# One load per token tile, with gate factor and token number carried through the tiles, in a fused attention, MoE and gated-MLP kernel

## The reference, cut to what matters

```python
def reference(**kwargs):
    attn_out = _attn_ref(**attn_kwargs)          # recurrent attention, (B, H, S, D)
    x = attn_out.transpose(0, 2, 1, 3).reshape(B * S, H * D)
    x = _moe_ref(x=x, **moe_kwargs)
    return _moe2_ref(x=x, **moe2_kwargs)

def _moe_ref(x, w_gate, w_output_gate, w1, w2):
    logits = x @ w_gate
    e_idx = np.argmax(logits, axis=1)            # one expert for each token
    ...
    for e in range(E):
        mask = e_idx == e
        h = np.maximum(x[mask] @ w1[e], 0.0)
        ye = h @ w2[e]
        out[mask] = gate_w[mask, None] * eom[mask, e, None] * ye
    return out

def _moe2_ref(x, w_gate, w_val, w_out, rms_g):
    xn = x / np.sqrt(np.mean(x * x, axis=-1, keepdims=True) + 1e-06) * rms_g
    g = xn @ w_gate
    return (g / (1.0 + np.exp(-g)) * (xn @ w_val)) @ w_out
```

## Time and profile before

| what | value |
|---|---|
| median of 3 runs | 879.19 us (878.07 to 881.12) |
| profiled execution, its own time | 886.08 us |
| its span | 884.3 us |
| PE busy | 822.9 us (93%) |
| DVE busy | 511.9 us (58%) |
| ACT busy | 387.7 us (44%) |
| POOL busy | 135.9 us (15%) |
| q1, the queue that SP issues to | 103.11 MB, 42.2% of 16 engines |
| DMA packets | 92492, of them 19464 under 512 B |

### The profile page before, as it was taken

The page is one execution under the profiler, slowest core; times in us unless marked ns, Lnnn a source line. Parts: engine busy times, 40 slices in busy tenths (PEclk is TensorE's granted clock), DMA queues, the critical chain, the costliest instruction groups (busy, mean ns, idle before and its releaser), DMA issues.

```text
span 884.3 us, 18262 instructions
## 1 busy us (share of the span) xinstructions
PE 822.9 (93%) x6219; PEld 739.2 (84%) x6219; DVE 511.9 (58%) x1060; ACT 387.7 (44%) x703; POOL 135.9 (15%) x196
## 2 busy tenths in 40 slices
PE   7999999509999999999989999999999999999994
PEld 4877777408999999999988888888888888888884
DVE  5388877647687868777774354344344344344331
ACT  5454544115777777677673233233233233233221
POOL 3467776510000000000000001001001001001001
PEclk8699999657999999999999999999999999999998
DMA  5577775189999999998980100100100100100000
GB/s 184 131 185 205 198 201 154 64 249 269 267 265 264 282 272 280 258 278 254 300 231 16 37 1 30 37 1 30 36 0 30 36 0 30 36 0 30 1 1 30
DMA packets 92492, 114.30 MB, mean 129 GB/s; under 512 B 19464, under 2 KB 71208, under 8 KB 92440
## 3 DMA queue, kind: packets, MB, share of 16 engines
q1 hardware_dynamic: 87960, 103.11, 42.2%
q0 software_dynamic: 2304, 7.89, 2.6%
q10 hardware_dynamic: 2176, 2.64, 1.0%
HBM read 97.18 MB, written 16.46 MB: 129 GB/s over the span
## 4 chain that ended last, share of the span: by engine, by line
PE 71%; POOL 10%; issue 8%; DVE 3%; SPq 2%; DMA 2%; ACT 1%; ACTq 1%; POOLq 0%; DVEq 0%
PE psum L1459 41%; PE psum L1534 5%; PE psum L1533 5%; PE psum L1532 5%; PE psum L1486 4%; PE psum L1487 4%; PE psum L1488 3%; POOL zT L643 3%; POOL prob_T L617 2%; POOL x_by_expert L652 2%; DMA w_raw<-w 1%; POOL v_weighted L627 1%; PE psum L1451 1%; PE psum L1511 1%; PE psum L1372 1%
## 5 line engine op out<-in xcount | busy, mean ns | idle before, releaser
L1285 DVE TENSOR_TENSOR gated_lo<-gated,gated_hi 128x512 fp32r<-128x512 f32 x72 | 49.8, 692 | 181.5 <-ACT gated_hi L847 170.5
L842 ACT ACTIVATE sigm_sb<-psum 128x512 f32<-128x512 f32 x72 | 43.1, 598 | 248.9 <-PE psum L1459 234.1
L681 POOL DMA_INDIRECT out<-out_rows,slot_idx x24 | 23.0, 959 | 669.7 <-ACT out_rows L853 664.2
L1459 PE MATMUL psum<-nT_hi,w_gv_hi 128*128 128x512 f32 x432 | 122.2, 391 | 1.8 <-DVE nT_lo L1272 1.8
L1459 PE MATMUL psum<-nT_lo,w_gv_hi 128*128 128x512 f32 x432 | 121.9, 390 | 0.0
L1459 PEld LDWEIGHTS psum<-nT_lo,w_gv_hi 128*128 128x128 f32 x432 | 81.1, 188 | 17.8
L1459 PEld LDWEIGHTS psum<-nT_hi,w_gv_hi 128*128 128x128 f32 x432 | 78.6, 188 | 14.4 <-issue 2.1
L1532 PE MATMUL psum<-w_out_hi,gated_hi 128*128 128x320 f32 x288 | 89.1, 309 | 0.0
L1534 PE MATMUL psum<-w_out_hi,gated_lo 128*128 128x320 f32 x288 | 89.0, 309 | 0.0
L1533 PE MATMUL psum<-w_out_lo,gated_hi 128*128 128x320 f32 x288 | 88.9, 309 | 0.0
L1459 PE MATMUL psum<-nT_hi,w_gv_lo 128*128 128x512 f32 x288 | 88.7, 389 | 0.0
(11 more groups left out here) (206 smaller groups left out, 1564.1 us busy)
## 6 DMA issues: line engine op xcount, KB each, us to landing
w_raw<-w SPq DMA_DIRECT2D x38, 640.0 KB, 7.4
w_raw<-w SPq DMA_DIRECT2D x38, 512.0 KB, 4.8
w_raw<-w SPq DMA_DIRECT2D x76, 128.0 KB, 5.6
kv_tok<-tok SPq DMA_DIRECT2D x24, 324.0 KB
qk_sb<-qk SPq DMA_DIRECT2D x48, 160.0 KB
y_sorted<-y_tile SPq DMA_DIRECT2D x12, 321.0 KB, 5.4
og_tok<-o_tok SPq DMA_DIRECT2D x24, 160.0 KB
x_tile<-x_by_expert SPq DMA_DIRECT2D x12, 320.0 KB, 2.9
```

Source lines behind the costliest of these rows:

```text
L842: nc.scalar.activation(sigm_sb[f % 2][:], bank[2 * (f % 2)][:], ACT.Sigmoid).then_inc(sig_ready, 1)
L1285: dve.tensor_tensor(gated_lo[f % 4][:], gated[f % 2][:], gated_hi[f % 4][:].bitcast(F32), ALU.subtract).then_inc(hv_lo, 1)
L1459: m = mm(dst, w, x, start=(n == 0), stop=(n == len(terms) - 1))
```

## The change

The rows of `x_by_expert` become 386 columns wide (`XW`): 320, the last 64 again, gate factor, token number. ScalarE makes the 64 doubled columns in `y_tok` with a new function `double_tail`, 24 copies of 128 x 64 in the attention stage; each scatter waits for it. The zero rows are 386 columns wide too. `x_load` is one transfer of whole rows. In the expert stage GpSimd runs a new function `keep_meta(j)` for each tile: it copies the two extra columns from `x_tile` to a small buffer `row_meta`, and from there to `y_tile`, which is 323 columns wide now. The store writes all 323 columns, the copy from DRAM to DRAM and one table read are gone, `x_load(j)` waits for `meta_kept`, and the store waits for `meta_moved`.

```diff
             def x_load(j, w):
                 row = sp.value_load(rowi[0:1, bass.ds(j, 1)], min_val=0, max_val=IDLE)
                 wait(sp, xt_made, j)
-                xr = x_by_expert[bass.ds(row, w), :].rearrange("(s p) n -> p s n", p=P)
-                sp.dma_start(x_tile[:, 0:w // P, 0:DM], xr[:, :, 0:DM]).then_inc(x_in, 16)
-                sp.dma_start(x_tile[:, 0:w // P, DM:KB * P], xr[:, :, DM - TAIL:DM]).then_inc(x_in, 16)
+                wait(sp, meta_kept, j)
+                sp.dma_start(x_tile[:, 0:w // P], x_by_expert[bass.ds(row, w), :].rearrange("(s p) n -> p s n", p=P)).then_inc(x_in, 16)
...
             def expert_store(j, w):
-                row = sp.value_load(rowi[0:1, bass.ds(j, 1)], min_val=0, max_val=IDLE)
                 to = sp.value_load(stori[0:1, bass.ds(j, 1)], min_val=0, max_val=NTOK)
                 wait(sp, e_stored, 16 * j)
-                wait(sp, meta_in, 16 * j)
                 sp.sem_inc(sync_turn, 1)
-                sp.dma_start(y_sorted[bass.ds(to, w), DM + 1:YW], x_by_expert[bass.ds(row, w), DM:XW]).then_inc(meta_in, 16)
+                sp.wait_ge(meta_moved, j + 1)
+                sp.sem_inc(sync_turn, 1)
                 sp.wait_ge(e_copied, 2 * j + 2)
                 sp.wait_ge(e_squared, 2 * j + 2)
                 sp.sem_inc(sync_turn, 1)
-                sp.dma_start(y_sorted[bass.ds(to, w), 0:DM + 1].rearrange("(s p) n -> p s n", p=P), y_tile[:, 0:w // P]).then_inc(e_stored, 16)
+                sp.dma_start(y_sorted[bass.ds(to, w), :].rearrange("(s p) n -> p s n", p=P), y_tile[:, 0:w // P]).then_inc(e_stored, 16)
...
+            def keep_meta(j, w):
+                n = w // P
+                pool.wait_ge(x_in, 16 * j + 16)
+                pool.sem_inc(pool_turn, 1)
+                pool.tensor_copy(row_meta[:, 0:n], x_tile[:, 0:n, KB * P:XW]).then_inc(meta_kept, 1)
+                pool.wait_ge(meta_kept, j + 1)
+                pool.sem_inc(pool_turn, 1)
+                wait(pool, e_stored, 16 * j)
+                pool.sem_inc(pool_turn, 1)
+                pool.tensor_copy(y_tile[:, 0:n, DM + 1:YW], row_meta[:, 0:n]).then_inc(meta_moved, 1)
+                pool.wait_ge(meta_moved, j + 1)
+                pool.sem_inc(pool_turn, 1)
...
+            def double_tail(n):
+                act.wait_ge(y_ready, n + 1)
+                nc.scalar.activation(y_tok[:, n % NY, DM:KB * P], y_tok[:, n % NY, DM - TAIL:DM], ACT.Copy).then_inc(tail_doubled, 1)
...
                 if i + 3 < NT:
                     gates(i + 3)
+                if i >= 3:
+                    double_tail(i - 3)
```

More of the change, by code:

```diff
@@ L67 @@
 NY = 12
-XW = DM + 2
+XW = KB * P + 2
 YW = DM + 3
@@ L187, in build @@
         second_lo = sb("second_lo", [P, NF1, DM], F32R, ge)
-        x_tile = sb("x_tile", [P, 2, KB * P], F32, ge)
+        x_tile = sb("x_tile", [P, 2, XW], F32, ge)
         xT_hi = sb("xT_hi", [P, KB, TE], F32R, ge)
@@ L192, in build @@
         hT_lo = sb("hT_lo", [P, NF1 // 2, 2 * TE], F32R, ge)
-        y_tile = sb("y_tile", [P, 2, DM + 1], F32, ge)
+        y_tile = sb("y_tile", [P, 2, YW], F32, ge)
+        row_meta = sb("row_meta", [P, 2, 2], F32, ge)
         squares = sb("squares", [P, DM], F32, ge)
@@ L285, in build @@
         store_rows = sem("store_rows")
-        meta_in = sem("meta_in")
+        tail_doubled = sem("tail_doubled")
+        meta_kept = sem("meta_kept")
+        meta_moved = sem("meta_moved")
         cnt_table = sem("cnt_table")
@@ L533, in _ @@
             sp.wait_ge(e_stored, 16 * FIRST_STORES)
-            sp.wait_ge(meta_in, 16 * FIRST_STORES)
             c_load(0)
@@ L541, in _ @@
             sp.wait_ge(e_stored, 16 * NTE)
-            sp.wait_ge(meta_in, 16 * NTE)
             with sp.Fori(1, NTC) as t:
@@ L650, in scatter @@
                 pool.wait_ge(ids_made, n // B + 1)
+                pool.wait_ge(tail_doubled, n + 1)
                 pool.sem_inc(pool_turn, 1)
@@ L674, in _ @@
                 scatter(n)
+            def keep_meta(j, w):
[10 more added lines that the diff above has]
+                pool.sem_inc(pool_turn, 1)
+            keep_meta(0, TE)
+            with pool.Fori(1, NFULL) as j:
+                keep_meta(j, TE)
+            with pool.Fori(NFULL, NTE) as j:
+                keep_meta(j, TS)
             def tokens(t):
@@ L752, in _ @@
                     gates(i + 3)
+                if i >= 3:
+                    double_tail(i - 3)
             outputs(NT - 1)
+            for n in range(NT - 3, NT):
+                double_tail(n)
             gate_exp(NC - 1)
@@ L1014, in gate_end @@
                         dve.wait_ge(scattered[n], 16)
-                dve.reciprocal(y_tok[:, slots, DM], gate_sum[:, 4]).then_inc(scale_ready, 1)
-                dve.tensor_copy(y_tok[:, slots, DM + 1], token_id[:, B * g:B * g + B]).then_inc(ids_made, 1)
+                dve.reciprocal(y_tok[:, slots, XW - 2], gate_sum[:, 4]).then_inc(scale_ready, 1)
+                dve.tensor_copy(y_tok[:, slots, XW - 1], token_id[:, B * g:B * g + B]).then_inc(ids_made, 1)
             def rank_read(g):
@@ L1445, in x_turn @@
             def x_turn(j, w):
-                pe.wait_ge(x_in, 32 * j + 32)
+                pe.wait_ge(x_in, 16 * j + 16)
                 wait(pe, x_lo, 2 * j)
```

## The result

| | before | after |
|---|---|---|
| median of 4 runs each, same chip | 879.71 us (878.07 to 881.12) | 905.33 us (900.97 to 913.48) |
| ratio, 95% interval | | 1.0275 [1.0228, 1.0321] |
| profiled execution, its own time | 886.08 us | 902.97 us |
| its span | 884.3 us | 901.2 us |

Ratios and their intervals come from fast executions alone and are not quotients of the medians printed beside them, so the two can differ in the third decimal. The ratio is 24 us on 879.7, with 20 to 28 for its interval. The forecast was +19.4 us. The single profiled executions differ by 17 us only, because what comes before the experts varies between executions; the next table takes that apart.

The account below looks back on a forecast made before the run. PE paces the full tiles, with DMA nearly as busy; SP and the queue bound the half tiles. Expert stage +17.6 and between stages +1.8 gave +19.4 us: 905.5 on the profiled 886.1, 898.6 on the median 879.2; range 886 to 908.

Parts of the forecast that it names:

- rival (b): Expert stage: slow way back from landed store to SP, stalls lowering PE's clock; rounds 16.5 and 15.2, 907.6 us; chance 0.10.
- The new wait: Expert stage: x_load(j) waits through GpSimd for the store issued just before it, so the queue drains once a tile.
- Full rounds: Full tiles, from one tile's first w1 load to the next: 15.9 us against PE's 15.37, ends 15.37 and 16.5.
- T(3): Issue of tile 3's first w1 load (T(j) is tile j's), where the full-tile count starts; forecast to move by 1.5 us.
- Half rounds: Half tiles, four rounds from tile 14 to 18: 14.6 us each against 11.8, +11.3 us in all.
- hidden(18) 12.6 us after T(18): Last half tile: hidden(18) begins 12.6 us after tile 18's first w1 load, at 478.3, +17.6 us.
- Between the stages: Between attention and experts: wider zero transfers and scatters, 0.65 MB more ahead of the wait, +1.8 us (0 to +3).
- Attention: Attention stage: ScalarE's 24 copies and the scatters' added 0.8 MB cost 0, upper end 1 us.
- Rival (a): Full tiles hide the wait, PE keeps 15.37 us and only half tiles pay: +13.6, 892.8 us; chance 0.21.
- (c): Rival, faster: the store lands early, no wait decides, SP's savings show in the half tiles: -4.7, 874.5 us; chance 0.08.
- (e): Rival: small packets are dear, so removing them hides the full tiles' wait; half rounds 13.5, +8.3, 887.5 us; chance 0.10.
- SP's savings buy nothing: Half tiles: SP saves some 1.3 us before the store's issue, without gain, since the store waits in the queue.

Follow-up runs that it names:

- e1: The changed kernel with two row_meta buffers and the copy made a tile ahead, so x_load waits for no store: 877.36 us, 0.9957 of the kernel before.
- e2: The kernel before with one wait added: x_load(j) waits on SP until the store of tile j-3 has landed: 894.16 us, ratio 1.0195.
- e5: The kernel before with the 8-byte DRAM to DRAM copy made twice, the second into another buffer: 884.13 us, ratio 1.0034.

## Why the prediction came out as it did

Forecast 898.6 us in 886 to 908, slower; the median is 905.33. It lies in the stated range, but just outside the forecast's own 893 to 904 and nearer to rival (b)'s 907.6. The mechanism is the one forecast. The half tiles' round and the step behind T(18) came out too small, and the stretch between the stages too large. The full tiles' round came out right by two errors that cancel, which is luck.

- **The new wait.** Right. In tile after tile x_load follows the landing of the store issued just before it, released by POOL (11 waits, 42.1 us in 215 to 395 us). It follows by 1.3 to 2.0 us from tile 4 on, and by 2.2 in tile 3, where I had written 0.7 to 1.5. e1 takes the wait away and all of the loss goes; e2 brings it back alone.
- **Full rounds** 15.9 forecast, 15.93 measured. T(3) moved by 1.1 (forecast 1.5) and T(14) by 7.7 (forecast 7.7), counted from the first matmul. The queue was drained at T + 13.6 on average (12.6 to 14.5, from each tile's store and its time to landing), beside 13.9 to 14.3 worked out, and the way from the landing to w1 took 2.4 us instead of 1.7; the two errors cancel. The 15.6 from which I worked was one tile's: the eleven stores before land between T + 14.1 and T + 15.7, at T + 14.8 on average. The way is longer than in the half tiles because GpSimd's two copies take 0.73 us together instead of 0.52.
- **Half rounds** 14.6 forecast, 15.5 measured: +15.0 us over four instead of +11.3. This is the mis-sized term. The drained time was 13.4 us (12.9, 13.9, 13.0 and 13.7) against 12.9: the 0.3 us that I took off for the 8-byte copy didn't show, and e2, which still has that copy, drained in about 13.0. The 13.2 that I started from was the mean of two tiles; with the next two, at 13.3 and 14.9, it is 13.6, so the base was read too low, but why e2 then drains earlier than after stays open. The way from landing to w1 was 2.1 us against 1.7. Of it SP's part was 0.7 (forecast 0.8). GpSimd's was 1.3 to 1.6 instead of 0.9, because the two copies stand 0.56 us apart, and the first takes 0.23 to 0.45 us and not 0.19.
- **hidden(18) 12.6 us after T(18).** It took 13.3 us (465.31 to 478.63). The chain of after between T(18) and hidden(18):

```profile
466.48 4.83 DMA w_raw<-w
...
472.72 0.65 ACT hT_hi L806 x2
...
474.82 0.44 DVE hT_lo L1225
...
475.39 0.60 PE psum L1513
```

PE had stood for 5.2 us when it went on at 475.39, and its last twelve matmuls ahead of hidden(18) took 3.24 us at a granted clock of 0.52. The 12.6 was read from tile 15 of before, where the same twelve took 1.84 us at a full clock:

```profile
422.27:424.11 1.84, 1.84 (x13) 1.84 (x14) 1.84 (x4) 1.37 (x2) 0.00 (x0) 1.00 1.03 294
475.39:478.63 3.24, 3.23 (x13) 3.24 (x13) 3.18 (x6) 2.51 (x4) 0.40 (x1) 0.52 0.49 162
```

So the lower clock costs 1.4 us here, more than the whole 0.7 by which the step was short; the forecast's own sum had put the clock at nothing. The start of hidden(18) before was misread too. Rows 5 show the last piece of the chain on PE, not the end of expert_out(17), which the timeline of before puts 0.7 us later:

```profile
461.23 0.31 PE L1488 MATMUL psum<-second_hi,hT_lo 128*128 128x320 f32 x1
461.37 0.45 PE L1459 MATMUL psum<-xT_hi,first_hi 128*128 128x128 f32 x3
```

From the first matmul hidden(18) therefore moved by 21.4 us (259.35 to 280.75), against +17.6 forecast, which is +16.9 from the right start. The last stage then began 21.0 late.

- **Between the stages** +1.8 us forecast, +0.9 measured over ten traces. I added the bytes at the stage's rate and took nothing off for transfers that lie beside others; that this is the reason is not shown.
- **Attention** 0 forecast. All counts are ready at 168.96 to 177.7 us in the ten traces, in 170.0 to 177.7 with the doubling on ScalarE and 168.96 to 176.73 without: no cost visible, and none under some 4 us could be.
- **The sum.** 21.0 + 0.9 = 21.9 us by the traces, against 19.4 forecast and 24 [20, 28] by the ratio. The other 2 us lie within the interval and are not placed.
- **Rival (a)** falls with the full rounds. **(b)** was half right: the way back is slower than taken, by 0.4 us in the half tiles and 0.7 in the full ones, in place of its 0.6, and the half rounds, 15.5, are longer than its 15.2. With the longer stalls the granted clock did fall, from 0.97 to 0.94 between hidden(14) and hidden(18), and the same 366 matmuls take 48.3 us instead of 45.8. The rounds don't show it, since SP's next loads wait for the store and for GpSimd and not for PE; the step behind T(18) does. **(c)** falls with landings of 6.0 to 8.3 us (its own numbers put the landing at which it would decide at 2.8 us, not 2.6). Yet the gain that it spoke of is real once the wait is gone: its sum was -4.7 us, and e1's ratio gives -3.8 (-6.7 to -0.9). **(e)** falls with the rounds, 15.5 and not 13.5 in the half tiles, and with e5, whose interval ends under its +8.
- I wrote that SP's savings buy nothing, since the store waits in the queue. That holds only with the wait, and it is the second half of the answer to where the change's merit went: after is 29.0 us of expert stage behind e1 by the traces, of which 21.0 show against before and 8.0 were the gain that it lost; by the two ratios it is 28 us of the whole time, of which 24 show.

## What to carry to other kernels

A semaphore that frees a buffer carries every wait that stands ahead of its increment on that engine: when a small copy is put on an idle engine, look at what the copy before it in the same list waits for, and who sits behind the one that waits on it. A store is last in a shared queue, so a loader that waits for its landing lets the queue run empty once a round, even where the engines looked bound by PE. Two small buffers and the copy one tile ahead, or only the order of two loads, turned 1.0275 into 0.9957 and 0.9973.

## What the runs showed of the hardware

**A tiny GpSimd copy can take five times its own time.** The copies of 128 x 4 take 0.19 us alone. The timeline of the kernel after around 226 us, where VectorE subtracts with both inputs in SBUF, and a little earlier, where its input comes from PSUM:

```profile
224.93 0.41 DVE L1204 TENSOR_TENSOR xT_lo<-psum,xT_hi 128x256 fp32r<-128x256 f32 x1
...
225.16 0.19 POOL L685 COPY y_tile<-row_meta 128x4 f32<-128x4 f32 x1 [22.52 <-DMA y_sorted<-y_tile]
...
225.70 1.23 DVE L1211 TENSOR_TENSOR first_lo<-w_raw,first_hi 128x1024 fp32r<-128x1024 f32 x1 [0.35 <-ACT first_hi L794]
...
225.91 1.06 POOL L680 COPY row_meta<-x_tile 128x4 f32<-128x4 f32 x1 [0.57 <-POOL y_tile L685]
```

Both end within 0.04 us of each other (226.93 and 226.97): the copy came second and was held until VectorE was done. Beside the operation that reads PSUM it was not held. The Trainium skill, page "SBUF — State Buffer", section "Who interferes with whom", says this of a VectorE instruction with two SBUF inputs against a GpSimd instruction that reads SBUF: they share a port, and the one that comes second blocks. This trace agrees. On the way back the two copies of a tile took 0.41 to 1.06 us together from tile 4 on, against 0.38 for two that run alone; the copy at 416.24, 0.39 us long, ran beside such subtractions. I take the excess for the same effect; it is not shown copy by copy.

**GpSimd's handover to itself.** Between the end of one copy and the start of the next, over the end of a loop with a wait for its own semaphore, lie 0.54 to 0.57 us in every tile of after, three times the copy. In e1, whose loop is written out, it is 0.26 us (403.41 + 0.29 = 403.70, and the next copy at 403.97):

```profile
403.41 0.29 POOL L688 COPY y_tile<-row_meta 128x2 f32<-128x2 f32 x1 [11.12 <-DMA y_sorted<-y_tile]
403.97 0.48 POOL L680 COPY row_meta<-x_tile 128x2 f32<-128x2 f32 x1 [0.26 <-POOL y_tile L688]
```

**Small packets.** The Trainium skill, page "DMA: Bandwidth & Descriptors", section Specifications, wants 512 B for full rate. The runs neither bear out a large price nor measure a small one: 3,968 packets of 8 B more changed the expert stage by 0.1 us in one trace, and the time by 3 us with an interval of -0.8 to +6.7 us.
